# First unit of the top-1 mixture: low-part products last, two low pieces of w2 on GpSimd, first layer's low part ahead of the plan on VectorE

## What is computed

```
logits = xn @ en.T / tau
expert_idx = argmax(logits, axis=1)
gate_w = softmax(logits)[expert_idx]
for e in range(E):                       # E = 8, D = 512, F = 1024
    h = maximum(x[mask] @ w1[e], 0.0)
    out[mask] = gate_w[mask, None] * (h @ w2[e])
```

## Time and profile before

| | us |
|---|---|
| median of 3 runs | 359.79 |
| lowest and highest | 358.73 and 361.72 |
| the profiled execution, its own time | 360.49 |
| its span, first to last instruction | 358.6 |
| mean granted TensorE clock | 0.955 |
| TensorE busy with matmuls | 325.7 (91%) |
| VectorE, ScalarE, GpSimd busy | 148.9, 145.3, 132.0 |

### The profile page before, as it was taken

The page is one execution under the profiler, slowest core; times in us unless marked ns, Lnnn a source line. Parts: engine busy times, 40 slices in busy tenths (PEclk is TensorE's granted clock), DMA queues, the critical chain, the costliest instruction groups (busy, mean ns, idle before and its releaser), DMA issues.

```text
span 358.6 us, 8871 instructions
## 1 busy us (share of the span) xinstructions
PE 325.7 (91%) x3484; PEld 245.5 (68%) x3485; DVE 148.9 (42%) x267; ACT 145.3 (41%) x249; POOL 132.0 (37%) x135
## 2 busy tenths in 40 slices
PE   5899999999999978999709889999999999999990
PEld 4688878786878843342403567888888888888870
DVE  2575666765676536140188952222022102211200
ACT  6455757664665631102024634344144414441310
POOL 6444443442454200010302355554455345533321
PEclk9599999999999999989957999999999999999997
DMA  8999999999786859999556302111111111111010
GB/s 217 295 332 341 311 350 339 331 319 339 233 243 231 285 202 383 388 387 385 153 164 246 140 19 75 46 66 67 46 47 63 50 60 44 66 39 59 33 63 31
DMA packets 57053, 67.15 MB, mean 187 GB/s; under 512 B 3160, under 2 KB 40360, under 8 KB 57008
## 3 DMA queue, kind: packets, MB, share of 16 engines
q1 hardware_dynamic: 52896, 56.97, 49.1%
q0 software_dynamic: 4096, 9.53, 7.8%
q10 hardware_dynamic: 16, 0.02, 0.0%
HBM read 58.64 MB, written 7.88 MB: 185 GB/s over the span
## 4 chain that ended last, share of the span: by engine, by line
PE 79%; DMA 8%; SPq 3%; DVE 3%; issue 2%; ACT 2%; POOL 1%; POOLq 0%; DVEq 0%
PE ps L1540 34%; PE psAB L1295 7%; PE psAB L1330 6%; DMA W<-in_moe_w_dram 5%; PE psAB L1388 4%; PE ps L1241 4%; PE ps L1319 3%; PE psAB L1337 3%; PE psAB L1531 3%; PE ps L1233 3%; PE ps L1257 3%; PE ps L1621 3%; SPq L400 2%; PE psAB L1249 2%; PE ps L1276 2%
## 5 line engine op out<-in xcount | busy, mean ns | idle before, releaser
L721 POOL TENSOR_TENSOR W<-W,cst 64x512 f32<-64x512 f32 x48 | 51.6, 1074 | 64.2 <-PE psAB L1295 57.3
L1113 DVE SCALAR_TENSOR_TENSOR h_low<-psAB,h_high 128x1024 fp32r<-128x1024 f32 x24 | 28.3, 1220 | 98.8 <-ACT h_high L632 98.7
L644 ACT ACTIVATE yout<-ps,gates 128x512 f32<-128x512 f32 x24 | 16.6, 690 | 89.1 <-PE ps L1540 73.4
L754 POOL DMA_INDIRECT out_dram<-yout,target x24 | 24.3, 1011 | 63.0 <-ACT yout L644 62.4
L1540 PE MATMUL ps<-w_high,h_high 128*128 x176 | 44.7, 396 | 0.0
L1540 PE MATMUL ps<-w_high,h_low 128*128 x176 | 43.6, 390 | 0.1
L1540 PE MATMUL ps<-w_low,h_high 128*128 x176 | 43.6, 389 | 0.0
L884 DVE TENSOR_TENSOR W<-psAB,cst 128x1024 f32<-128x1024 f32 x24 | 29.4, 1224 | 21.4 <-PE psAB L1295 21.4
L1540 PEld LDWEIGHTS ps<-w_high,h_low 128*128 128x128 f32 x176 | 33.0, 188 | 7.3 <-issue 0.5
L1540 PEld LDWEIGHTS ps<-w_low,h_high 128*128 128x128 f32 x176 | 33.0, 188 | 7.1
L1540 PEld LDWEIGHTS ps<-w_high,h_high 128*128 128x128 f32 x176 | 32.2, 188 | 6.6 <-issue 0.3
(11 more groups left out here) (242 smaller groups left out, 459.2 us busy)
## 6 DMA issues: line engine op xcount, KB each, us to landing
W<-in_moe_w_dram SPq DMA_DIRECT2D x40, 512.0 KB, 6.9
W<-in_moe_w_dram SPq DMA_DIRECT2D x6, 2048.0 KB, 13.9
W<-in_k_dram SPq DMA_DIRECT2D x12, 512.0 KB, 5.6
W<-in_q_dram SPq DMA_DIRECT2D x12, 512.0 KB, 6.1
W<-in_v_dram SPq DMA_DIRECT2D x12, 512.0 KB, 7.4
W<-in_moe_w_dram SPq DMA_DIRECT2D x2, 1024.0 KB, 6.1
w_raw<-in_moe_w_dram SPq DMA_DIRECT2D x4, 512.0 KB, 8.0
token_rows<-rows POOLq DMA_DIRECT2D x4, 384.0 KB, 4.6
```

What stands on the lines that cost most here:

```text
L721: nc.gpsimd.tensor_tensor(ks[n % 3].rearrange("p (h d) -> p h d", h=H)[odd * P // 2:(odd + 1) * P // 2], of_chunk(k_raw2, n, odd), fac, AL ...
L754: nc.gpsimd.indirect_dma_start(out=out, out_offset=bass.IndirectOffsetOnAxis(ap=target[:, WT * i + v:WT * i + v + 1], axis=0), in_=yout[v] ...
L1113: V.scalar_tensor_tensor(h_low[u][:, part_of], psAB[:, part_of], 0.0, h_high[u][:, part_of].bitcast(fp32), ALU.max, ALU.subtract).then_inc ...
```

## The change

On VectorE the gates come first, then `split_h(0, 0)`, the targets and low piece 3, and the plan behind them in one go. Low pieces 1 and 2 are made by GpSimd with a `tensor_tensor` of 128 partitions x 1024 each, behind the DMA of the gates; GpSimd's wait for the targets, `load_gates(0, v)` and `load_rows(2)` follow them. On TensorE the order becomes: 12 products `h_high x w_high` (pieces 0 to 2), `transpose_s(1)`, 12 products with `h_low` (pieces 0 to 2, both v), the 4 + 4 products of piece 3, 8 products with `w_low` for v = 0, the plan, `hidden(1, 1)`, 8 products with `w_low` for v = 1, `transpose_s(2)`, and then the loop. The number of products and of VectorE's and GpSimd's DMAs and small instructions is the same.

```diff
--- before.py
+++ after.py
@@ -265,7 +265,7 @@
             sem(n) for n in ("sw_ready", "sw_copied", "sum_ready", "s_high", "s_ready"))
         c_ready, cT_ready, cT_all_copied = sem("c_ready"), sem("cT_ready"), sem("cT_all_copied")
         rhs_q_ready, q_ready, q_compared, q_read = (sem(n) for n in ("rhs_q_ready", "q_ready", "q_compared", "q_read"))
-        high_act, high_dve = sem("high_act"), sem("high_dve")
+        high_act, high_dve, low_pool = sem("high_act"), sem("high_dve"), sem("low_pool")
         low_made, targets_ready = sem("low_made"), sem("targets_ready")
         squared, norm_ready, shift_ready, exp_ready, gate_ready, gate_out = (
             sem(n) for n in ("squared", "norm_ready", "shift_ready", "exp_ready", "gate_ready", "gate_out"))
@@ -789,14 +789,22 @@
             load_rows(0)
             pool.wait_ge(sT_ready, 1)
             load_rows(1)
-            pool.wait_ge(targets_ready, 1)
             pool.wait_ge(gate_ready, 1)
             pool.dma_start(token_gates.rearrange("(p n) o -> p (n o)", p=P), gate[:, :]).then_inc(gate_out, 16)
-            pool.wait_ge(sT_ready, 2)
-            load_rows(2)
+            for c in range(1, PIECES - 1):
+                if c == 1:
+                    pool.wait_ge(high_dve, 1)
+                else:
+                    pool.wait_ge(high_act, c)
+                part_of = slice(c * SLOT // PIECES, (c + 1) * SLOT // PIECES)
+                nc.gpsimd.tensor_tensor(w_low[:, part_of], w_raw[:, part_of], w_high[:, part_of].bitcast(fp32), ALU.subtract
+                                        ).then_inc(low_pool, 1)
+            pool.wait_ge(targets_ready, 1)
             pool.wait_ge(gate_out, 16)
             for v in range(WT):
                 load_gates(0, v)
+            pool.wait_ge(sT_ready, 2)
+            load_rows(2)
             pool.wait_ge(sT_ready, 3)
             load_rows(3)
             pool.wait_ge(plan_ready, 1)
@@ -1087,10 +1095,7 @@
 
             def low_piece(c):
 
-                if c == 1:
-                    dve.wait_ge(high_dve, 1)
-                else:
-                    dve.wait_ge(high_act, c + 1 if c < 1 else c)
+                dve.wait_ge(high_act, max(c, 1))
                 part_of = slice(c * SLOT // PIECES, (c + 1) * SLOT // PIECES)
                 return V.tensor_tensor(w_low[:, part_of], w_raw[:, part_of], w_high[:, part_of].bitcast(fp32), ALU.subtract)
 
@@ -1148,15 +1153,17 @@
             V.tensor_copy(w_high[:, SLOT // PIECES:2 * SLOT // PIECES], w_raw[:, SLOT // PIECES:2 * SLOT // PIECES]
                           ).then_inc(high_dve, 1)
             low_piece(0).then_inc(low_made, 1)
+            dve.wait_ge(exp_ready, 1)
+            done(V.tensor_reduce(gate[:, :].rearrange("p (g r) -> p r g", r=4), by_bank(lg[:, :], e=E), AX.X, ALU.add))
+            done(V.tensor_scalar(gate[:, :], gate[:, :], 1e-9, None, ALU.add))
+            V.reciprocal(gate[:, :], gate[:, :]).then_inc(gate_ready, 1)
+
+            split_h(0, 0)
             done(V.tensor_scalar(beyond, in_tile, 1.0, float(2 * NT * P), ALU.is_lt, ALU.mult))
             V.scalar_tensor_tensor(target[:, :], in_token, -float(P), beyond, ALU.add, ALU.add)
             done(V.scalar_tensor_tensor(in_lane, in_lane, float(NT), in_tile, ALU.mult, ALU.add))
             V.tensor_scalar(gate_row[:, :], in_lane, -1.0, 0.0, ALU.add, ALU.max).then_inc(targets_ready, 1)
-
-            dve.wait_ge(exp_ready, 1)
-            done(V.tensor_reduce(gate[:, :].rearrange("p (g r) -> p r g", r=4), by_bank(lg[:, :], e=E), AX.X, ALU.add))
-            done(V.tensor_scalar(gate[:, :], gate[:, :], 1e-9, None, ALU.add))
-            V.reciprocal(gate[:, :], gate[:, :]).then_inc(gate_ready, 1)
+            low_piece(PIECES - 1).then_inc(w2b_split, 1)
 
             done(V.tensor_scalar(has, cnt, 1.0, None, ALU.min))
             done(V.tensor_tensor_scan(hinc, onesn[:, 0:E], has, 0.0, ALU.mult, ALU.add))
@@ -1169,7 +1176,6 @@
             V.tensor_copy(tei[:, TB + 2:TB + 1 + E], uex[:, 1:E])
             V.tensor_copy(tei[:, TB + 1 + E:TB + 2 + E], hinc[:, E - 1:E]).then_inc(experts_ready, 1)
 
-            low_piece(1).then_inc(low_made, 1)
             done(V.tensor_scalar(last_place[:, :], hinc[:, E - 1:E], -1.0, None, ALU.add))
             done(V.tensor_scalar(tinc, tinc, 1.0 / (WT * P), None, ALU.mult))
             ce = part[:, 0:TB * E].rearrange("p (i e) -> p i e", i=TB)
@@ -1188,10 +1194,6 @@
             done(V.tensor_scalar(tef[:, 1:TB], tef[:, 1:TB], 1.0, None, ALU.add))
             V.scalar_tensor_tensor(nexti[:, 1:TB].unsqueeze(2), ce[:, 1:TB, 0:1], float(NEVER), tef[:, 1:TB].unsqueeze(2),
                                    ALU.mult, ALU.add).then_inc(plan_ready, 1)
-
-            low_piece(2).then_inc(low_made, 1)
-            low_piece(PIECES - 1).then_inc(w2b_split, 1)
-            split_h(0, 0)
 
             dve.wait_ge(plan_ready, 1)
             live = dve.value_load(n_used, min_val=1, max_val=E)
@@ -1621,30 +1623,45 @@
                 return mm((psU, psY)[v][:, :], of_tile(h, v)[:, j, :], w[:, j * DM:(j + 1) * DM], **flags)
 
             per = KF // PIECES
-            for c in range(PIECES):
+
+            def first_high(c):
                 if c == 1:
                     pe.wait_ge(high_dve, 1)
                 else:
-                    pe.wait_ge(high_act, c + 1 if c < 1 else c)
+                    pe.wait_ge(high_act, max(c, 1))
                 for v in range(WT):
                     for j in range(c * per, (c + 1) * per):
                         if v == 0 and j % (KF // 2) == 0:
                             pe.wait_ge(relu_done, j // (KF // 2) + 1)
                         first_product(v, h_high[0], w_high, j, start=(j == 0), stop=False)
-            transpose_s(1)
-            for c in range(PIECES):
-                if c < PIECES - 1:
-                    pe.wait_ge(low_made, c + 1)
-                else:
-                    pe.wait_ge(w2b_split, 1)
+
+            def first_rest(c):
                 for v in range(WT):
                     for j in range(c * per, (c + 1) * per):
-                        first_product(v, h_high[0], w_low, j, start=False, stop=False)
-            for j in range(KF):
-                if j % (KF // 2) == 0:
-                    pe.wait_ge(h_low_ready, j // (KF // 2) + 1)
-                last = first_product(0, h_low[0], w_high, j, start=False, stop=(j == KF - 1))
-            last.then_inc(z_ready, 1)
+                        if v == 0 and j % (KF // 2) == 0:
+                            pe.wait_ge(h_low_ready, j // (KF // 2) + 1)
+                        first_product(v, h_low[0], w_high, j, start=False, stop=False)
+
+            def first_low(v):
+                for j in range(KF):
+                    if v == 0 and j % per == 0:
+                        if j == 0:
+                            pe.wait_ge(low_made, 1)
+                        elif j < KF - per:
+                            pe.wait_ge(low_pool, j // per)
+                        else:
+                            pe.wait_ge(w2b_split, 1)
+                    last = first_product(v, h_high[0], w_low, j, start=False, stop=(j == KF - 1))
+                last.then_inc(z_ready, 1)
+
+            for c in range(PIECES - 1):
+                first_high(c)
+            transpose_s(1)
+            for c in range(PIECES - 1):
+                first_rest(c)
+            first_high(PIECES - 1)
+            first_rest(PIECES - 1)
+            first_low(0)
             pe.wait_ge(plan_ready, 1)
             live_experts = pe.value_load(n_used, min_val=1, max_val=E)
             live_tiles = pe.value_load(n_tiles, min_val=TF, max_val=TB)
@@ -1656,12 +1673,9 @@
                     fold(2)
                     sum_fold(2)
                     pe.wait_ge(s_ready, 4)
-            pe.wait_ge(sT_copied, 2)
+            hidden(1, 1)
+            first_low(1)
             transpose_s(2)
-            hidden(1, 1)
-            for j in range(KF):
-                last = first_product(1, h_low[0], w_high, j, start=False, stop=(j == KF - 1))
-            last.then_inc(z_ready, 1)
 
             def extra(i):
                 with pe.If(live_tiles > i):
```

## The result

The changed kernel took 365.13 us (median of 6 runs, 363.92 to 367.32), the kernel before 361.39 (6 runs, 358.73 to 363.39, the three of the first table among them). The ratio is 1.0095, with a 95% interval of 1.0055 to 1.0135: 3.4 us slower (the two medians alone differ by 3.7). The profiled execution took 365.75 us, its span is 364.0, 5.4 more than before.

What follows compares the result with a forecast made beforehand. TensorE bounds the kernel: its loop has fixed length, so its start sets the end. A loop start 3.75 us later plus 1.7 us for the clock gave +5.5 us on 359.79, so 365.3 us; range 360.4 to 367.5.

Steps and rivals of the forecast that it cites:

- its own parts: Chances of over 1% slower: the forecast 0.55, half of rival 2, and rival 4 with 0.07; given as 0.66.
- The loop's start sets the end: TensorE's loop over units 1 to 11 has fixed length; its start, 216.30 us, moves the end by as much.
- The hold on VectorE: VectorE's targets, reading two SBUF tensors, stand still until GpSimd's two 2.1 us instructions end; VectorE resumes at 206.9.
- rival 4: GpSimd's instructions take 3.0 us each, pushing the plan by 1.8 us more: 367.1 us; chance 0.07.
- The plan: On VectorE, 4.14 us in one go behind low piece 3, ready at 212.7 us.
- Plan to `stage`: ScalarE's register loads and branches take 3.16 us from plan to start of `stage`, 4.22 us to its end.
- Rival 3: The 3.16 us before `stage` shrink during a longer wait; loop 1.2 us earlier, 358.6 us; chance 0.08.
- TensorE's gain of 1.4 us, not collected: TensorE is ready for `hidden(1, 1)` at 212.0 instead of 213.41, but `stage` is finished only at 216.9.
- The clock: TensorE's 5.7 us gap lowers its clock; 3.4 to 3.8 us at the lower level lose 1.7 us.
- Rival 2: VectorE is held but TensorE's clock stays up: +3.75 us, 363.5 us; chance 0.1.
- Rival 1: VectorE isn't held or takes every turn: loop +0.75 us, up to +2.5 if the clock falls; chance 0.2.
- the slack of the plan: Between VectorE's plan and TensorE's use of `stage` at 213.41 us, 2.7 us of slack, said to decide the change.

Runs made afterwards that it cites:

- e2: The changed kernel with 20 full fp32 products that nobody uses on TensorE before the wait for the plan; 374.18 us, 1.0361 of the kernel before.
- f3: The changed kernel, but GpSimd waits for its first subtraction to complete before issuing the second; one run only, plan ready at 11.38 us instead of 11.64.
- f4: The changed kernel measured again, unaltered; 365.91 us or 365.57 us (order not stated), 1.0155 of the kernel before.
- g2: The changed kernel measured once more, unaltered; 1.0120 of the kernel before (1.0077 to 1.0163).
- f1: The changed kernel with 6 full fp32 products that nobody uses filling TensorE's gap before the plan; 1.0150 of the kernel before.
- g1: The changed kernel with the same 6 unused products in TensorE's gap as f1, measured again; 1.0039 of the kernel before.
- e1: The changed kernel, but low pieces 1 and 2 are made on VectorE behind the plan, none on GpSimd; 1.0073 of the kernel before.
- e4: Against the changed kernel: VectorE makes the plan right behind low piece 0 and the gates, GpSimd makes no pieces, TensorE reordered; 1.0084 of the kernel before.

## Why the prediction was right, point by point

- **The time, and some luck in it.** Forecast 365.3, measured 365.13: nearer than the forecast had earned. What it forecast was a rise of 5.5 us over 359.79; the rise was 3.4 us (2.0 to 4.9 by the interval, which 5.5 is outside of), over a kernel before that now stood at 361.39. The two errors, some 2 us too much rise and 1.6 us too low a start, nearly cancelled. The two later measurements, 5.6 and 4.3 us, have 5.5 inside their intervals; the mean of the three is 4.5. And 1.0095 is just under the 1% that the forecast had put at chance 0.66 to be passed (its own parts, 0.55, 0.05 and 0.07, make 0.67).
- **The loop's start sets the end.** Right in the main: e2 moved both by 9 us. Forecast: 3.75 + 1.7 = 5.45 us later (the terms as given add up to 220.01 for the loop, not 220.05); the traces show 5.6, 6.1 and 6.1 for the start, but 5.1 to 5.4 for the end, since the loop of the kernel before was 0.5 to 0.8 us longer, which the forecast had put at nothing.
- **The hold on VectorE.** The mechanism was right and carried the forecast. GpSimd's instruction was a little mis-sized: 2.39 us instead of 2.1, so rival 4, with 3.0, is out. That VectorE would get in between the two was wrong in the detail: the two ran through, for 3.43 us; f3 shows that a queued second instruction is what keeps it out, and that the detail costs 0.3 us at most. The instruction that was held has one input tensor in SBUF, where the forecast looked for the hold on the two that read two. The end of the hold, forecast at 206.85, was 207.1. The estimate from the table of the Trainium skill, "GPSIMD Engine Reference", section 3.1, was 2.25 us for one instruction; the measured 2.39 is nearer to it than to my 2.1.
- **The plan.** Forecast at 212.7, ready at 212.94 in an execution that began the unit 0.32 us later.
- **Plan to `stage`.** Taken as fixed at 3.16 us; it was 3.15 to 3.16 in every kernel of the table, whether the plan was early or 6 us late. Rival 3, which needed it to shrink, is out.
- **TensorE's gain of 1.4 us, not collected.** Right: its last product of v = 0 ended at 210.9, and it waited 6.33 us, against the 5.7 forecast.
- **The clock.** Forecast 1.7 us, from 3.4 to 3.8 us at the lower level; measured 1.95 in the trace (2.2 in f4 and g2), since the lower level lasted 4.3 us from TensorE's return; the earlier trace rows show 3.8 busy us at that level, and the 3.4 stands in no row. The times of f1 and g1 against f4 and g2 gave about 1.6, too uncertain to settle it. Rival 2 is out: the clock fell in all three profiled executions of the changed kernel.
- **Rival 1** (VectorE not held) is what e1 shows with the pieces taken away: the loop 1.0 us later, where I had worked out 0.75.

What a reader could weigh from the profile of before alone is thus the slack of the plan, 2.7 us, against the work put ahead of it: 3.45 us by e1 (8.94 - 5.49; I had worked out 3.2), and the hold added 2.7 more (11.64 - 8.94; I had 3.0).

## What to carry to other kernels

Before work is moved to GpSimd beside a chain of small VectorE instructions, ask what that chain is doing meanwhile: two subtractions of 2.4 us held a 38-column instruction for 3.43 us, and in another order a 64-column one for 5.30. `split_h`, which has an input in PSUM, kept its 2.35 us beside the same pair, so that is the kind to put there. And before a step is put ahead of another on a queue, work out the slack of what moves back, up to its last user on the other engines; here a plan of tiny instructions had 2.7 us of slack and came 6.15 us later, and the gap then cost again through the clock.

## What the runs showed of the hardware that I had not expected

- Two queued GpSimd instructions keep a waiting VectorE instruction out over both (3.43 us, and 4.13 where it came 0.7 us earlier), even one with a single input tensor in SBUF; with a wait between them it gets in after the first (1.07 us).
- The clock was at its lower level for 6.8 us around the gap in the changed kernel (214.8 to 221.6), 4.3 of them after TensorE had come back to work.
- GpSimd's issue of an indirect DMA, mostly 0.94 to 1.02 us, took 1.72 us beside VectorE's low piece 3, and 1.54 and 1.96 beside low pieces in e4. But two issues beside the same instruction in the kernel before took 0.97 and 1.02 (206.13 and 207.41), so what decides it is open.
- A product of full fp32 operands with 512 columns takes 0.84 us where the rounded type takes 0.23 to 0.25.
